# Two more unread 512-column products behind each fold of the search rounds (gated scan and two mixtures of experts, one core)

## What is computed

```python
def _moe_ref(x, w_gate, w1, w2):
    logits = x @ w_gate
    order = np.argsort(-logits.flatten())
    for idx in order:                      # greedy, in the order of all logits
        tok, e = int(idx) // E, int(idx) % E
        if assigned[tok] >= 0 or counts[e] >= cap:
            continue
        assigned[tok] = e; counts[e] += 1
    ...
    out[mask] = np.maximum(x[mask] @ w1[e], 0.0) @ w2[e]

def _moe2_ref(x, expert_emb, tau, w1, w2):
    xn = x / (norm(x) + 1e-6); en = expert_emb / (norm(expert_emb) + 1e-6)
    logits = xn @ en.T / tau
    expert_idx = np.argmax(logits, axis=1)
    ...
    out[mask] = gate_w[mask, None] * (np.maximum(x[mask] @ w1[e], 0.0) @ w2[e])
```

## Time and profile before

| | us |
|---|---|
| median of three timed runs | 1464.65 |
| the three runs | 1464.65, 1465.47, 1461.06 |
| the profiled execution | 1465.98 |
| its span, first to last instruction | 1464.5 |
| its mean granted clock | 0.905 |
| TensorE busy | 1286.9 (88% of the span) |
| VectorE busy | 838.4 (57%) |
| ScalarE busy | 728.7 (50%) |
| GpSimd busy | 464.5 (32%) |

### The profile page before, as it was taken

One profiled execution on the slowest core, in us unless ns is written; L12 is line 12 of the kernel. 1 busy time (PEld: TensorE's weight loads), 2 busy tenths in 40 slices (PEclk: granted clock), 3 DMA queues, 4 the chain that ended last, 5 costly groups with the idle time before them and its releaser, 6 DMA issues. The chain is left out here.

```text
span 1464.5 us, 28375 instructions
## 1 busy us (share of the span) xinstructions
PE 1286.9 (88%) x9338; PEld 1196.4 (82%) x9340; DVE 838.4 (57%) x2271; ACT 728.7 (50%) x1347; POOL 464.5 (32%) x585
## 2 busy tenths in 40 slices
PE   3656657887599999999999999489999999999997
PEld 3655656666259999999999999479999999999997
DVE  5778777666746665665666666534335444435332
ACT  5555644455327675666666666334334344334332
POOL 3344530000034444443444444322222222222222
PEclk9788766566779999999999999789999999999999
DMA  6566732210021231222223221252213331311111
GB/s 216 184 180 210 228 120 83 87 58 30 1 79 59 74 101 41 101 70 69 72 73 102 73 73 44 72 177 76 70 39 98 102 106 48 98 43 42 43 43 43
DMA packets 81201, 129.16 MB, mean 88 GB/s; under 512 B 7974, under 2 KB 63919, under 8 KB 81104
## 3 DMA queue, kind: packets, MB, share of 16 engines
q1 hardware_dynamic: 62448, 74.10, 15.9%
q0 software_dynamic: 18656, 53.81, 11.6%
HBM read 94.61 MB, written 35.10 MB: 89 GB/s over the span
## 5 line engine op out<-in xcount | busy, mean ns | idle before, releaser
L972 PE MATMUL ps<-xTh,w1h 128*128 128x256 f32 x1312 | 376.4, 287 | 5.3 <-issue 3.5
L976 PE MATMUL ps<-xTl,w1h 128*128 128x256 f32 x1312 | 372.9, 284 | 0.2 <-issue 0.2
L973 PE MATMUL ps<-xTh,w1l 128*128 128x256 f32 x1312 | 372.8, 284 | 0.0
L1569 DVE SCALAR_TENSOR_TENSOR hidl<-ps,hidh 128x512 fp32r<-128x512 f32 x328 | 225.7, 690 | 230.5 <-ACT hidh L696 221.8
L696 ACT ACTIVATE hidh<-ps 128x512 fp32r<-128x512 f32 x328 | 195.5, 596 | 250.9 <-PE ps L976 242.3
L972 PEld LDWEIGHTS ps<-xTh,w1h 128*128 128x128 f32 x1312 | 252.5, 192 | 6.3 <-issue 3.9
L973 PEld LDWEIGHTS ps<-xTh,w1l 128*128 128x128 f32 x1312 | 252.8, 193 | 1.7
L976 PEld LDWEIGHTS ps<-xTl,w1h 128*128 128x128 f32 x1312 | 253.0, 193 | 0.4 <-issue 0.4
L1009 PE MATMUL ps<-w2hl,hidh 128*128 128x512 f32 x672 | 239.9, 400 | 0.0
L993 PE MATMUL ps<-w2hl,hidh 128*128 128x264 f32 x640 | 185.1, 289 | 0.0
L995 PE MATMUL ps<-w2hl,hidl 128*128 128x264 f32 x640 | 182.1, 285 | 0.0
(11 more groups left out here) (280 smaller groups left out, 2266.7 us busy)
## 6 DMA issues: line engine op xcount, KB each, us to landing
w1st<-in_moe_w_dram SPq DMA_DIRECT2D x20, 1024.0 KB, 5.5
w2st<-in_moe_w_dram SPq DMA_DIRECT2D x19, 1024.0 KB, 5.5
xrow<-y_rows POOLq DMA_DIRECT2D x44, 258.0 KB
arena<-in_r_gate_dram SPq DMA_DIRECT2D x19, 512.0 KB, 4.8
arena<-in_i_gate_dram SPq DMA_DIRECT2D x19, 512.0 KB, 5.9
arena<-in_x_dram SPq DMA_DIRECT2D x19, 512.0 KB, 6.7
h_rows<-w2st POOLq DMA_DIRECT2D x19, 512.0 KB, 4.2
y_rows<-arena SPq DMA_DIRECT2D x8, 258.0 KB, 2.7
```

Source lines behind the costliest of these rows:

```text
L972: pe.matmul(o, wh, xTh[:, hf, :], start=(hf == 0), stop=False)
L973: pe.matmul(o, wl, xTh[:, hf, :], start=False, stop=False)
L976: mm = pe.matmul(o, wh, xTl[:, hf, :], start=False, stop=(hf == HB - 1))
L1569: dve.scalar_tensor_tensor(out=hidl[:, 2 * fp:2 * fp + 2, :].rearrange("p c t -> p (c t)"), in0=bank(fp), scalar=0.0, in1=hidh[:, 2 * fp:2 ...
```

## The change

```diff
@@ -905,6 +905,7 @@
                         fold_turn(n)
                     if 2 <= n < FOLDS + 2:
                         fold_dots(n - 2)
+                        keep_busy(2, 1)
                     elif n >= FOLDS + 2:
                         keep_busy(5)
             pe.wait_ge(floor_made, PASSES)
```

## The result

The changed kernel takes 1486.38 us (median; 1485.57 to 1486.66), the one before 1464.59 us. The ratio is 1.0153, with a 95% interval of 1.0135 to 1.017. The forecast was slower, 1478 us in a range of 1465 to 1485: right in its direction and in what happens in the search, and 1.4 us outside its range. The first mixture's 5.7 us had no term in it.

The account below looks back on a forecast made before the run. VectorE and ScalarE bound the search's fold rounds at 2.4 GHz, TensorE at 1.2 GHz. Exposed pairs +17.0 us less 3.7 us for longer high clock gave +13.3 us on 1464.65: 1478 us, range 1465 to 1485.

Parts of the forecast that it names:

- What bounds the search, and what a pair costs: Fold rounds: VectorE and ScalarE bound at 2.4 GHz, TensorE at 1.2 GHz; a pair costs 0 or 0.85 us, 20 exposed, +17.0 us.
- the 0.14 us that the prediction had left: Fold rounds at 2.4 GHz: a pair of 0.45 us fits TensorE's 0.59 us idle time before `count`, 0.14 us to spare.
- nothing in the keep rounds at 1.2 GHz: Rounds 5, 13, 21, 29, where ScalarE keeps folded columns: TensorE's 2.04 us idle time covers the pair, cost 0.
- VectorE's wait at the end of a pass: Last round of a pass at 1.2 GHz: the floor's transpose comes 0.85 us later, VectorE waits 3.1 us instead of 2.26.
- What the clock does: Search passes: the clock outlives the keep round nowhere or by one ordinary round, and does not rise again within a pass.
- one more ordinary round at 2.4 GHz: One such round in each of the second to fourth pass, 2.15 in place of 3.38 us: 3.7 us less in all.
- the sum: Whole change: +17.0 us for exposed pairs, less 3.7 us for longer high clock, +13.3 us, ends +9.6 and +17.0.
- nothing is removed or moved: The fold rounds' code: the change only adds two 512-column products in each of 32 rounds, 64 in all.
- 3 us for everything behind the search: After the search: 3 us added on either side, for run spread and later work starting elsewhere relative to the clock's steps.
- That the clock holds with two a round: Rival, fold rounds: two products keep 2.4 GHz through the keep round, 13.6 us faster, 1451 us; chance 0.13.

Follow-up runs that it names:

- The best version: Three wide products in every search round from 0 to 33, six in the keep rounds, against the kernel before: 1452.69 us, ratio 0.9931.

## Why the prediction was wrong, point by point

**What bounds the search, and what a pair costs: right.** 0.85 us a pair at 1.2 GHz (3.38 us a round), nothing at 2.4 GHz (rounds 8 and 16 still take 2.14 us; the room is larger than the 0.14 us that the prediction had left, as three products fit too), nothing in the keep rounds at 1.2 GHz (4.71 us before and after; the idle time shrank to 1.19 us as forecast), VectorE's wait at the end of a pass 3.04 us (3.1 forecast), 241 wide products.

**What the clock does: right in kind, off in one pass.** Forecast was one more ordinary round at 2.4 GHz in each of the second to fourth pass, worth 3.7 us. It came in the second and third: the round behind the keep round takes 2.28 and 2.16 us in place of 2.56. In the fourth the clock fell earlier in the pass, at 337.6 us, so that the whole keep round ran at 1.2 GHz and took 4.72 in place of 3.54 us; in the run with 16 small products more it did not. Against that, the ends of the four passes cost 2.1 us together and not 3.4, since the clock's rise in the ten products shifted too. From the `same_half` of a pass's first round to that of the next pass's it is +4.0, +3.1, +2.4 and +4.9 us, and +0.1 in the last pass: 14.6 us before rounding, where the sum had 13.3 with ends of 9.6 and 17.0. By this part alone the median would have been 1479 us.

**The step that failed: "nothing is removed or moved", and 3 us for everything behind the search.** The sum priced 64 products by where they stand in time, and not the 128 instructions by where they put the code behind them. That cost 5.7 us in the first mixture. Without it the changed kernel would lie at about 1481 us, within the range; the run in which 16 small products take the second wait out gave 1478.14 us. That this is the forecast to 0.2 us is luck, as the kernel before took 1465.89 us beside it and two falls of the clock were absent. The trace of before had the sign of it in the waits for "issue" at each turn of the loop (1.79 us at 555.02), but not the size: the second wait was absent there and is absent at most other places. It came with 128 instructions more, in three kernels with different work in them (the change, small products in idle time, narrow products in the rounds), and not with 64, 160, 192, 224, 252, 256 or 272 more. The two parts, 14.6 and 5.7 us, make 20.3 us, which is just what lies between the two profiled executions (1486.25 and 1465.98). The medians are 21.8 us apart; the other 1.5 us are, for the most part, that the profiled execution of the kernel before took 1.4 us more than its median.

What falls at that place is argued, not seen. The runs show that the number of instructions ahead decides on the second wait; that it is the border of two fetched pieces fits them, but no view says with which instruction a piece begins, and no run moved the wait to another product of the loop.

**The rivals.** That the clock holds with two a round was worth 13.6 us in the forecast. The mechanism is real. Its place was named rightly only in part. The prediction put it at the idle time of the keep rounds, but its own rows have the clock fall at 268.9 us, and the 1.25 us of idle time in that keep round begin at 269.62; in the changed kernel the clock fell 1.2 and 1.8 us behind the first keep round of the second and third pass, and ahead of it in the fourth. Two products don't reach it; with the keep rounds filled or with four everywhere it came. The best version, with the clock up in all but a few rounds, brings 11.7 us. The Trainium skill, page "TensorE: Matmul & The Clock Gate", section "Why this matters for your kernels", advises against long idle gaps between bursts of matmuls, as they make the clock drop. By that it should hold in the fold rounds, which have no long ones. This is not borne out: after the change the clock fell at 276.1 us with no idle time above 1.26 us in the 10.2 us before, and then TensorE was 95% busy for 23.8 us at 1.2 GHz and the clock did not rise.

## What to carry to other kernels

Filler work is not priced by its own length but by which side of the clock it ends up on: here one, two and three products a round each cost time and four save it, so try the amount until the clock holds. Filling the longest idle time first is worth a try: eight products there and two elsewhere gave 1459.7 us, four in each of these rounds 1458.9 us with 16 products more. Fill no more than the round holds at 2.4 GHz (here three products were free, and the fourth cost 0.1 us a round). And in a kernel with loops, compare the stages that weren't touched as well: instructions added anywhere ahead of a loop can put a wait for code into it, and a few more, in idle time, can take it out again.

## What the runs showed of the hardware that I had not expected

- A wait of 2.21 to 2.53 us, for code by all that the runs show, in the middle of a run of products, seven products behind a jump back. It came and went with how many instructions stand ahead of it, whatever work they did. It came at both jumps back of the loop in the first mixture, and made the block there 16.4 to 17.3 us long in place of 12.34 to 13.84.
- The first wait at the same jump (1.33 to 2.15 us) was there in every execution read, and the clock can drop to 1.2 GHz for some 3.4 us at or behind it although TensorE is dense on both sides. That is 1.5 us a turn, and may be a part of the 4 us by which executions of one kernel differ.
- At 1.2 GHz fold rounds with two more wide products keep TensorE 95% busy by the profile, and the clock stays down; at 2.4 GHz rounds with the same work and visible idle time kept it up between filled keep rounds. Busy time in the profile did not tell which way it goes.
